# Gated attention and two expert layers on one core: attention as one 16-step pipeline with regrouped matmuls

## The reference, cut to what matters

```python
# q, k, v: (2, 8, 768, 64)
gamma = 1.0 - 2.0 ** (-5.0 - np.arange(H)); scale = 1.0 / np.sqrt(D)
for t in range(S):
    state = gamma[None, :, None, None] * state + np.einsum('bhd,bhe->bhde', k[:, :, t], v[:, :, t])
    y[:, :, t] = scale * np.einsum('bhd,bhde->bhe', q[:, :, t], state)
x = y.transpose(0, 2, 1, 3).reshape(B * S, H * D)          # (1536, 512)
# layer 0 (moe_): rows with x @ w_skip > 0 get x + gate * relu(x @ w1[e]) @ w2[e], e = argmax(x @ w_gate)
# layer 1 (moe2_): rows get gate * relu(x @ w1[e]) @ w2[e], up to 384 rows per expert, the others zero
```

## Time and profile before

| | us |
|---|---|
| time of three runs: median (all) | 448.39 (452.54, 448.39, 447.13) |
| the profiled execution: span from first to last instruction | 447.1 |
| mean granted TensorE clock | 0.946 |
| attention, from the first instruction to the copy of batch 1's logits | 0 to 87.5 |
| layer 0: routing, experts, scatter | 87.5 to 229.5 |
| layer 1 | 229.5 to 447.1 |

### The profile page before, as it was taken

One profiled execution on the slowest core, in us unless ns is written; L12 is line 12 of the kernel. 1 busy time (PEld: TensorE's weight loads), 2 busy tenths in 40 slices (PEclk: granted clock), 3 DMA queues, 4 the chain that ended last, 5 costly groups with the idle time before them and its releaser, 6 DMA issues.

```text
span 447.1 us, 7645 instructions
## 1 busy us (share of the span) xinstructions
PE 398.9 (89%) x2818; PEld 351.0 (78%) x2818; DVE 217.3 (49%) x294; ACT 162.9 (36%) x180; POOL 118.0 (26%) x153
## 2 busy tenths in 40 slices
PE   3999999848999999999815699999999999999991
PEld 3777777637999999899714598989898989898981
DVE  1754565380425552355218346474737374646430
ACT  1112212231433544254103444554545464646410
POOL 4542332151033322321115200505050505050100
PEclk9999999956999999999955699999999999999998
DMA  8998999611999989989830244848585757750100
GB/s 257 372 335 293 317 386 369 220 23 43 333 322 310 346 309 327 322 305 306 299 114 12 85 134 158 273 179 273 188 252 206 248 201 218 236 165 19 46 12 20
DMA packets 58371, 98.73 MB, mean 221 GB/s; under 512 B 7404, under 2 KB 21740, under 8 KB 58352
## 3 DMA queue, kind: packets, MB, share of 16 engines
q1 hardware_dynamic: 52064, 84.14, 56.5%
q0 software_dynamic: 4736, 14.29, 9.1%
q10 hardware_dynamic: 1552, 0.05, 0.2%
HBM read 87.38 MB, written 12.67 MB: 224 GB/s over the span
## 4 chain that ended last, share of the span: by engine, by line
PE 84%; DMA 6%; DVE 3%; issue 3%; POOL 1%; ACT 1%; SPq 0%; POOLq 0%; DVEq 0%
PE ps_h L973 32%; PE ps_y L999 26%; PE ps_o L906 4%; PE ps_o L903 3%; PE ps_s L876 3%; PE ps_t L944 3%; PE ps_l L918 3%; PE ps_u L888 3%; PE ps_y L1014 2%; DMA xg<-x_rows,slot_id 2%; DMA xg<-x_rows,g_idx 1%; PE ps_g L1031 1%; PE ps_r L927 1%; DVE slots L758 1%; DMA k_in<-in_k_rows 1%
## 5 line engine op out<-in xcount | busy, mean ns | idle before, releaser
L783 DVE TENSOR_TENSOR w_lo<-raw,w_hi 128x2048 fp32r<-128x2048 f32 x48 | 109.0, 2287 | 49.8 <-ACT w_hi L576 49.8
L576 ACT CAST w_hi<-raw 128x2048 fp32r<-128x2048 f32 x48 | 90.4, 1904 | 14.2 <-issue 11.3
L794 DVE SCALAR_TENSOR_TENSOR h_lo<-ps_h,h_hi 128x512 fp32r<-128x512 f32 x48 | 33.1, 690 | 94.1 <-ACT h_hi L585 94.1
L999 PE MATMUL ps_y<-w_hi,h_hi 128*128 128x512 f32 x176 | 70.6, 401 | 0.0
L999 PE MATMUL ps_y<-w_lo,h_hi 128*128 128x512 f32 x176 | 68.7, 390 | 0.0
L999 PE MATMUL ps_y<-w_hi,h_lo 128*128 128x512 f32 x176 | 68.7, 390 | 0.0
L585 ACT ACTIVATE h_hi<-ps_h 128x512 fp32r<-128x512 f32 x48 | 28.7, 598 | 93.8 <-PE ps_h L973 93.8
L973 PE MATMUL ps_h<-x_f,raw 128*128 128x128 f32 x512 | 62.1, 282 | 0.7 <-ACT x_f L581 0.7
L973 PEld LDWEIGHTS ps_h<-x_f,raw 128*128 128x128 f32 x512 | 61.2, 198 | 1.6 <-ACT x_f L581 1.1
L474 POOL COPY g_idx<-slot_id 128x1 int32 (+1 forms) x12 | 13.0, 1086 | 157.9 <-ACT yo L605 102.2
L973 PE MATMUL ps_h<-x_hi,w_hi 128*128 128x256 f32 x256 | 41.4, 285 | 1.1 <-ACT x_hi L581 1.1
(11 more groups left out here) (101 smaller groups left out, 435.0 us busy)
## 6 DMA issues: line engine op xcount, KB each, us to landing
raw<-in_moe_w SPq DMA_DIRECT2D x64, 1024.0 KB, 5.8
q_t<-in_q_cols SPq DMA_DIRECT2D x16, 192.0 KB, 5.7
k_t<-in_k_cols SPq DMA_DIRECT2D x16, 192.0 KB, 5.4
k_in<-in_k_rows SPq DMA_DIRECT2D x16, 192.0 KB, 5.4
v_in<-in_v_rows SPq DMA_DIRECT2D x16, 192.0 KB, 5.4
out<-zero POOLq DMA_DIRECT2D x4, 768.0 KB, 7.4
x_rows<-rows SPq DMA_DIRECT2D x16, 192.0 KB, 4.3
table<-in_consts SPq DMA_DIRECT2D x1, 640.0 KB, 6.3
```

The lines of the kernel that those rows point to most:

```text
L576: nc.scalar.copy(w_hi[c], raw[:, 4 * job.par + c, :]).then_inc(hi_done[c], 1)
L783: nc.vector.tensor_tensor(w_lo[c], raw[:, 4 * job.par + c, :], w_hi[c].bitcast(F32), ALU.subtract).then_inc(lo_done[c], 1)
L794: nc.vector.scalar_tensor_tensor(out=h_lo[:, cols], in0=ps_h[:, g % 2, :], scalar=0.0, in1=h_hi[:, cols].bitcast(F32), op0=ALU.max, op1=AL ...
L999: last = pe.matmul(ps_y[:, t, :], ht, wt, start=(fb == 0 and z == 0), stop=(fb == 2 * QB - 1 and z == 2))
```

## The change

- The two turns of the loop become one straight sequence of 16 steps on every engine. The order within a batch is now `hp = n % 4`, half `n % 8 // 4`: first the first halves of all four pairs, then the second halves. `state` keeps four pairs.
- `outputs` is split. `past_outputs` does all state matmuls of a step in one go; PE's order in turn s is scores(s), updates(s), past_outputs(s-1), turn_rows(s-2), outputs(s-1).
- `turn_rows` multiplies `o_t` by `iw`, the identity beside `wr` (128 + 17 columns), in 3 matmuls that take the place of 3 transposes and 3 logit matmuls. ACT copies the 17 columns of each chunk into `lg_parts` and the rest into `rows`; DVE adds the four pairs' parts (`sum_logits`), once in four steps. `ps_l` is gone.
- Stores of rows are 8 of 384 KB instead of 16 of 192 KB. The table comes in five parts, one pair's at a time, and the identity is loaded four times, beside each pair's `wr`.
- SP waits for `o_done(n + 1)` before batch 1's loads and for `o_done(n)` before the chunks of weights, which begin at step 9 instead of 5 (steps 9 to 16).
- The output: POOL clears rows 0 to 63 at the start in four small DMAs; ACT clears the rest (2.9 MB) in two DMAs after layer 0, right behind the read of the logits. Every scatter of layer 1 first waits for `out_cleared`.

```diff
-FIRST_WEIGHTS = 5
+FIRST_WEIGHTS = 9
+STEPS = B * 2 * HP
...
-            for b in range(B):
-                for m in range(2 * HP):
-                    n = 2 * HP * b + m
-                    sp.wait_ge(rows_copied, n + 2)
...
-                    if FIRST_WEIGHTS <= n < FIRST_WEIGHTS + 8:
-                        load_chunk(...)
-                    if b == 0:
-                        sp.wait_ge(k_dec_done, n + 1)
-                        load_cols(1, m)
-                        load_rows(1, m)
-            sp.wait_ge(logits_copied, B + 1)
+            for n in range(STEPS + 1):
+                if n < 2 * HP:
+                    sp.wait_ge(o_done, n + 1)
+                    load_cols(1, n)
+                    load_rows(1, n)
+                if n >= 2 and n % 2 == 0:
+                    sp.wait_ge(rows_copied, n)
+                    store_rows(n - 1)
+                if FIRST_WEIGHTS <= n < FIRST_WEIGHTS + 8:
+                    sp.wait_ge(o_done, min(n, STEPS))
+                    load_chunk(...)
+            sp.wait_ge(logits_copied, 2 * B)
...
+            for z in range(4):
+                rows_z = slice(z * P // 8, (z + 1) * P // 8)
+                pool.dma_start(out[rows_z, :], zero[rows_z, 0:DM]).then_inc(yo_free[1][z % 2], 16)
...
-                    if m % 4 == 3:
-                        part = out.rearrange("(z g p) d -> z p g d", z=4, p=P)[bass.ds(2 * b + m // 4, 1)]
-                        pool.dma_start(part.rearrange("o p g d -> p (o g) d"), repeat(zero[:, 0:DM], 1, G // 4)
-                                       ).then_inc(yo_free[1][m // 4], 16)
...
+                    if i == 1:
+                        hold(pool, out_cleared, 32)
...
+            def copy_rows(n):
+                b, half, hp, k = n // (2 * HP), n % (2 * HP) // HP, n % HP, n // HP
+                both = ps_r[:, 0:HC * (P + NL)].rearrange("p (c w) -> p c w", c=HC)
+                act.wait_ge(rows_done, n + 1)
+                if hp == 0 and k >= 2:
+                    act.wait_ge(logits_copied, k - 1)
+                nc.scalar.copy(lg_parts[:, k % 2, hp], both[:, :, P:]).then_inc(parts_copied, 1)
+                act.wait_ge(rows_stored[2 * half + hp // 2], b * 16 + 16)
+                nc.scalar.copy(rows[:, half, :, hp * P:(hp + 1) * P], both[:, :, 0:P]).then_inc(rows_copied, 1)
+            for s in range(1, STEPS + 2):
+                if s >= 2:
+                    copy_rows(s - 2)
+                if s <= STEPS:
+                    copy_o(s - 1)
...
+                    act.dma_start(out[P // 2:P, :], zero[P // 2:P, 0:DM]).then_inc(out_cleared, 16)
+                    act.dma_start(out[P:N, :].rearrange("(g p) d -> p g d", p=P), repeat(zero[:, 0:DM], 1, G - 1)
+                                  ).then_inc(out_cleared, 16)
...
+            def sum_logits(k):
+                dve.wait_ge(parts_copied, HP * k + HP)
+                nc.vector.tensor_reduce(logits[:, k * HC:(k + 1) * HC, :].rearrange("p c n -> p (c n)"),
+                                        lg_parts[:, k % 2].rearrange("p h c n -> p (c n) h"), AX_X, ALU.add
+                                        ).then_inc(logits_copied, 1)
+            for n in range(STEPS):
+                decay_q(n)
+                mask(n)
+                states(n, chain)
+                if n % HP == 2 and n > HP:
+                    sum_logits(n // HP - 1)
+            sum_logits(2 * B - 1)
...
+            def past_outputs(n):
+                p, hp, c0 = n % 2, n % HP, (n % (2 * HP) // HP) * HC
+                pe.wait_ge(q_dec_done, n + 1)
+                pe.wait_ge(states_done, n + 1)
+                if n >= 1:
+                    pe.wait_ge(o_copied, n)
+                first = 1 if c0 == 0 else 0
+                for c in range(first, HC):
+                    pe.matmul(ps_o[:, c * P:(c + 1) * P], state[:, hp, c0 + c, :], q_dec[:, p, c, :],
+                              start=c == first, stop=False, skip_group_check=True)
...
+            def turn_rows(n):
+                pe.wait_ge(o_copied, n + 1)
...
                 for c in range(HC):
-                    last = pe.matmul(ps_l[:, (c0 + c) * NL:(c0 + c + 1) * NL], o_t[:, p, c * P:(c + 1) * P], wr[:, hp, :],
-                                     start=(m == 0 and c == 0), stop=(hp == HP - 1), skip_group_check=True)
...
-                for c in range(HC):
-                    last = pe.transpose(ps_r[:, c * P:(c + 1) * P], o_t[:, p, c * P:(c + 1) * P], ident)
+                    last = pe.matmul(ps_r[:, c * (P + NL):(c + 1) * (P + NL)], o_t[:, n % 2, c * P:(c + 1) * P], iw[:, n % HP, :],
+                                     start=True, stop=True)
                 last.then_inc(rows_done, 1)
-            with pe.Fori(0, B) as b:
-                for s in range(2 * HP + 2):
-                    for stage, m in ((scores, s), (updates, s), (outputs, s - 1), (turn_rows, s - 2)):
-                        if 0 <= m < 2 * HP:
-                            stage(b, m)
+            for s in range(STEPS + 2):
+                if s < STEPS:
+                    scores(s)
+                    updates(s)
+                if 1 <= s <= STEPS:
+                    past_outputs(s - 1)
+                if s >= 2:
+                    turn_rows(s - 2)
+                if 1 <= s <= STEPS:
+                    outputs(s - 1)
```

More of the change, by code:

```diff
@@ L55 @@
 NCONST = _at
-TABLE_CUTS = (0, _COLS["pair1"][0], _COLS["before"][0], NCONST)
+NTABLE = _COLS["ident"][0]
+TABLE_CUTS = (0, *(_COLS[f"pair{hp}"][0] for hp in range(1, HP)), _COLS["before"][0], NTABLE)
 def repeat(x, dim, n):
@@ L194, in program @@
         ps_g = ps("ps_g", [P, 512], ctx)
-        table_in = [sem(f"table_in{i}") for i in range(3)]
+        table_in = [sem(f"table_in{i}") for i in range(HP + 1)]
         wr_in = sem("wr_in")
+        ident_in = sem("ident_in")
         cap_in = sem("cap_in")
@@ L221, in program @@
         lg2_in = sem("lg2_in")
+        out_cleared = sem("out_cleared")
         state_link = sem("state_link")
@@ L355, in load_table, with store_rows @@
                 sp.dma_start(table[:, cols], consts[:, cols]).then_inc(table_in[i], 16)
+            def store_rows(n):
+                b, half, pair = n // (2 * HP), n % (2 * HP) // HP, n % HP // 2
+                t0, cols = b * S + half * HC * P, slice(pair * 2 * P, (pair + 1) * 2 * P)
+                sp.dma_start(x[t0:t0 + HC * P, cols].rearrange("(c p) d -> p c d", p=P),
+                             rows[:, half, :, cols]).then_inc(rows_stored[2 * half + pair], 16)
             def load_chunk(layer, job, c):
@@ L895, in outputs @@
                 pe.wait_ge(q_dec_done, n + 1)
                 pe.wait_ge(states_done, n + 1)
-                if m >= 1:
+                if n >= 1:
                     pe.wait_ge(o_copied, n)
-                for c in range(HC):
-                    cols = slice(c * P, (c + 1) * P)
-                    past = c0 + c > 0
-                    if past:
-                        pe.matmul(ps_o[:, cols], state[:, hp % 2, c0 + c, :], q_dec[:, p, c, :], start=True, stop=False,
-                                  skip_group_check=True)
+                first = 1 if c0 == 0 else 0
@@ L905, in outputs @@
+                for c in range(first, HC):
+                    pe.matmul(ps_o[:, c * P:(c + 1) * P], state[:, hp, c0 + c, :], q_dec[:, p, c, :],
+                              start=c == first, stop=False, skip_group_check=True)
+            def outputs(n):
+                p, hp, c0 = n % 2, n % HP, (n % (2 * HP) // HP) * HC
+                pe.wait_ge(probs_done, n + 1)
+                for c in range(HC):
                     for a in range(2):
-                        last = pe.matmul(ps_o[a * D:(a + 1) * D, cols], v_in[:, hp, c0 + c, a, :], probs[:, p, a, c, :],
-                                         start=not past, stop=True, skip_group_check=True)
+                        last = pe.matmul(ps_o[a * D:(a + 1) * D, c * P:(c + 1) * P], v_in[:, hp, c0 + c, a, :], probs[:, p, a, c, :],
+                                         start=False, stop=True, skip_group_check=True)
@@ L1030, in fin_route @@
                     for kk in range(KD):
-                        last = pe.matmul(ps_g[:, 0:E], e_t[:, kk, :], wr[:, kk, 1 + E:], start=(kk == 0), stop=(kk == KD - 1))
+                        last = pe.matmul(ps_g[:, 0:E], e_t[:, kk, :], iw[:, kk, P + 1 + E:], start=(kk == 0), stop=(kk == KD - 1))
                     last.then_inc(fin_logits, 1)
```

167 lines of the change are left out of this document (66 added, 101 removed).

## The result

The changed kernel takes 435.37 us (median of 4 runs, 434.73 to 435.88) against 447.91 for the kernel before: a ratio of 0.9694, 95% interval 0.9635 to 0.9753. The forecast was 432.7, in a range of 428 to 440. The span of the profiled execution went from 447.1 to 433.6 us, where the forecast had 431.4. In every execution on record the time is 1.6 to 1.9 us above its own span (here 435.46 and 433.6), the kernel before included; the 1.3 us between its median and the span 447.1 compares different executions.

What follows compares the result with a forecast made beforehand. PE was taken to bound the attention, losing time to changes of weight form. The attention's end moves from 87.75 to 72.1, so 447.1 - 15.7 = 431.4 us profiled and 432.7 for a median 1.3 above; range 428 to 440.

Steps and rivals of the forecast that it cites:

- changes of form: PE's attention step: each switch of weight form costs 0.16 to 0.2 us; eight become three, 1.0 us of a step.
- the twelve probs records: PE's attention step: the probs matmuls in one go take 0.6 us, within bounds of 0.6 to 1.1.
- the idle 0.17 us: PE's attention step: an idle PEld of 0.17 us stands before each row that follows a record of another form.
- the former seam: Between batch 0 and batch 1 in the attention: the drain and fill there now are gone after the change.
- The logits' sum: DVE in the attention: one reduction of 204 elements, between 0.24 and 0.56 us, once in four steps.
- ACT's extra copy: ACT in the attention step: one more copy of 153 elements from PSUM, 0 to 0.48 us, taken as 0.3.
- The end of the attention: Start of routing's reduction L731: at 72.1 us instead of 87.75, a gain of 15.7 us.
- Clears, loads, stores: Transfers at the start, in the attention and between layers: cost 0, up to 3 us if the queue is behind.
- the top row: Start of routing's first reduction, the end of the attention: forecast at 72.1 us, 87.75 before.
- rival (B): Attention: the transfers bound it, ending 2 to 3 us after the gather is due; 3 to 4 less gain, 436; chance 0.10.
- (A): PE's step: idle time comes with operand pairs, or long groups expose DVE or PSUM; 7 us less gain, 439.7; chance 0.14.
- (C): Between the layers: clears land 27 us later and hold the gathers, 15.7 us lost, 449 to 453; chance 0.03.

Runs made afterwards that it cites:

- turn_last: The changed kernel with turn_rows behind the probs matmuls instead of between state and probs, four changes of weight form in a step instead of three: 438.68 us.
- by_chunk: The changed kernel with state and probs matmuls interleaved by chunk again, as in the kernel before, behind turn_rows: 444.60 us.
- before_grouped: The kernel before with the regrouping alone, state matmuls ahead of turn_rows and probs matmuls behind it, still two turns of eight steps: 437.95 us.
- unfused: The changed kernel with rows and logits from 3 transposes and 3 matmuls of 17 columns again, without the matmul of 145 columns: 436.38 us.
- weights_7: The changed kernel with FIRST_WEIGHTS = 7, the chunks of weights in steps 7 to 14 instead of 9 to 16: 431.23 us.

## Why the prediction was right, and where it was off

**The mechanism.** The step came out as worked out, part by part: 3.95 us for 3.94, with the changes of form at 0.17 to 0.20 (0.16 to 0.2 read from the earlier trace rows), the twelve probs records at 0.63 for 0.6, turn_rows at 0.77 for 0.75. `turn_last` and `by_chunk` show the price of a change of form apart from everything else: the same matmuls with 3, 4 and 7 changes gave steps of 3.73, 3.93 and 4.42 us. The 1.10 us between the old step and the new are 0.89 for five changes (`before_grouped`) and 0.2 for the joint matmul (`unfused`). The Trainium skill (TensorEngine Tiling (Array Packing), Key Properties) says that changing the tiling mode drains the engine. The trace agrees that such a change costs time, 0.17 to 0.20 us each; that it is a draining that takes it, no row shows.

One reading of the earlier trace rows is too wide: the idle 0.17 us do not stand before each row that follows another form. The rows at 25.60 and 26.69 do follow another form and have none; there a change shows only in the distance of the starts, as the prediction worked it out for state to probs (0.43 us where two records take 0.22). And no gap is left at the former seam: from 25.98 to 63.26 no step of the changed kernel is longer than 3.95 us.

**DVE and ACT.** They kept up. The logits' sum took 0.50 us, in the upper half of 0.24 to 0.56, ACT's extra copy 0.20 for 0.3, and q_dec was never what PE waited for.

**The end of the attention.** 72.74 for 72.1. What I left out is a wait in step s = 16: with no scores and updates ahead of them its state matmuls wait for ACT's copy of `ps_o`, 0.7 us (67.0 to 67.7), which in every other step is covered:

```profile
66.18 0.63 PEld L927 LDWEIGHTS ps_o<-probs,v_in 128*64 128x64 f32 x12
...
67.11 0.48 ACT L561 COPY o_t<-ps_o 128x384 f32<-128x384 f32 x1 [0.23 <-PE ps_o L927]
...
67.70 0.74 PEld L919 LDWEIGHTS ps_o<-q_dec,state 128*128 128x128 f32 x6 [0.88 <-issue]
```

**The step that failed** is the end of "Clears, loads, stores": "A chunk lands in 5.8 us, at 78; the gather is due at 96.19 - 15.7 = 80.5. So 2 us to spare, cost 0, and up to 3 if the queue is behind." The sum took the 0. The 5.8 us are the median of all 64 chunks of the program; the eight beside the attention took 7.6 in the median and up to 11.5 in the same trace, and 9.8 at most in the changed kernel. And the same paragraph had 25.5 MB in 70 us, the full rate, which leaves nothing to spare. The backlog was there: the store landed at 82.5 and the gather came 3.4 us later than it was due (11.86 against 8.44 after the top row). That is rival (B) in its place, POOL's gather held by a landing, and the measured 435.4 is nearer to (B)'s 436 than to the forecast's 432.7. But it is not (B)'s reason: the engines' rate was not too low, they were at a share of 0.39 at 50 us for want of an issued chunk. `weights_7` shows that, with the same bytes, 394 GB/s at 50 us and no wait. So it is chance that (B)'s end of the transfers, 82.5, was met to the tenth.

**How the parts add up** in the span, against 431.4: top row +0.6; gather late +3.4, of which the gather's own two transfers gave back 1.2 (first turned rows at 89.08, 12.8 us earlier than before); layer 0 from there to its last turning 119.2 for 119.8, -0.6; between the layers -0.3, in which the clears' 0.7 are made up by a shorter scatter; layer 1 +0.2. Sum 2.1 to 2.2, to 433.6. Of the 0.6 us that layer 0 took less, 0.5 are a shorter wait of PE for one later gather:

```profile
189.06 0.66 PE L944 MATMUL ps_t<-table,xg 128*128 128x128 f32 x4 [0.77 <-DMA xg<-x_rows,g_idx]
```

before, and in the changed kernel

```profile
190.10 0.66 PE L963 MATMUL ps_t<-iw,xg 128*128 128x128 f32 x4 [0.28 <-DMA xg<-x_rows,g_idx]
```

The other kernels have 118.5 to 120.5 us there, so such a half microsecond is within what layer 0 varies by. The remaining 0.5 us of the 2.7 lies outside: the profiled execution took 435.46, 1.9 us more than its span, where I had taken the median as 1.3 above it; around every span on record lie 1.6 to 1.9 us. (The prediction also numbers the slices with 114, 12 and 85 GB/s as 20 to 22; they are 21 to 23, which changes nothing.)

**The other rivals.** (A) fell with `turn_last`. (C) is decided by the rows: the clears landed 9.4 us after their issue, not 27, before the gather; the stretch beside them is 0.5 to 0.7 us longer than without them. The rule by which a core has about 358 GB/s (DMA: Bandwidth & Descriptors, Specifications, in the Trainium skill) does not bound this kernel, and the measurement decides: `weights_7` moved 394 GB/s from 50 to 55 us.

## What to carry to other kernels

Read PE's pace from the starts of its weight loads: an engine that is busy at nine tenths can still lose nearly a fifth of a step (0.89 of 5.05 us) to changes of weight form, and the order of the same matmuls gives that back. When a stage gets shorter, look at what its transfers had to spare: loads that wait for the stage's steps end with it, and a small store that everything waits for then lands behind them. So start deferred bulk loads as soon as the engines have room, and keep the last microseconds before such a store empty.

## What was not expected of the hardware

- A store of 48 KB landed after 2.9 us in the kernel before, where the engines had been at a share of 0.10 from 86 to 88 us, after 4.2 in `weights_7`, and after 9.2 with some 2 MB in flight in the changed kernel (326 GB/s from 75 to 80 us), from SP's queue and from ACT's alike (9.2 and 9.1). The Trainium skill (DMA: Bandwidth & Descriptors, Issuing engines are not separate DMA queues) says that an issuing engine more saves only the time to issue; the trace agrees.
- PE's start of the slot matmuls in layer 1 is 0.86 us after DVE's last slots when the clears are flowing, 0.14 in the kernel before. What PE does there is read the number of windows into a register; that this read is what the transfers slow down was not tried by itself.
- Where the store was late, a longer PE stage was not passed on one to one. The first turned rows of layer 0 came 8.5 us later for 10.5 in `by_chunk` and 0.8 for 2.9 in `unfused`, but 2.2 for 1.9 in `turn_last`, where the store took 9.6 us instead of 9.2.
